# Order of ScalarE's copies and sines, and of VectorE's products, in a gated token mixer

## The reference, cut to what matters

```python
# attention: q, k, v, f_logit are [4, 8, 768, 48]
state = f[:, :, t, :, None] * state + k[t] outer v[t];  y[t] = q[t] @ state
# first mixer: x is [4, 768, 384]
theta = x @ w_theta
zr = x * cos(theta);  zi = x * sin(theta)
y = einsum('ts,bsd->btd', w_tok_r, zr) + einsum('ts,bsd->btd', w_tok_i, zi)
u = x + y
x2 = u + maximum(u @ w_ch, 0)
# second mixer
h = maximum(x2 @ w_in, 0);  u, v = halves of h;  v_n = normalised v
out = (u * (w_spatial @ v_n + b_spatial)) @ w_out
```

## Time and profile before

| | us |
|---|---|
| median of 3 executions | 602.97 |
| lowest, highest | 602.34, 603.02 |
| the profiled execution | 602.97 |
| its span, first to last instruction | 601.0 |
| PE busy | 574.9 (96%) |
| DVE busy | 366.5 (61%) |
| ACT busy | 290.1 (48%) |

### The profile page before, as it was taken

The page is one execution under the profiler, slowest core; times in us unless marked ns, Lnnn a source line. Parts: engine busy times, 40 slices in busy tenths (PEclk is TensorE's granted clock), DMA queues, the critical chain, the costliest instruction groups (busy, mean ns, idle before and its releaser), DMA issues.

```text
span 601.0 us, 11881 instructions
## 1 busy us (share of the span) xinstructions
PE 574.9 (96%) x4226; PEld 554.1 (92%) x4226; DVE 366.5 (61%) x614; ACT 290.1 (48%) x509; POOL 35.9 (6%) x66
## 2 busy tenths in 40 slices
PE   0898999999999999999999999999999999999997
PEld 0787888899999999999999999999999999999996
DVE  6899999777695557446754686556055705570250
ACT  5699999666553334424443536125222522262111
POOL 3223333100000000000000000000000000000000
PEclk9999999999999999999999999999999999999999
DMA  8988989477011230112023550200120010001102
GB/s 169 206 237 255 254 254 301 127 248 253 13 40 41 67 97 35 63 58 75 13 106 104 238 172 2 79 1 1 65 93 1 0 52 26 1 1 40 39 1 81
DMA packets 31113, 58.74 MB, mean 98 GB/s; under 512 B 3680, under 2 KB 23136, under 8 KB 30688
## 3 DMA queue, kind: packets, MB, share of 16 engines
q1 hardware_dynamic: 31072, 58.21, 31.7%
HBM read 44.04 MB, written 14.16 MB: 97 GB/s over the span
## 4 chain that ended last, share of the span: by engine, by line
PE 74%; DVE 3%; issue 2%; ACT 1%; DVEq 0%; ACTq 0%
PE gate_ps L1074 17%; PE theta_bank L1074 11%; PE ringc L1074 11%; PE small_ps L1074 10%; PE mix_ps L1540 8%; PE mix_ps L1545 8%; PE mix_ps L1541 8%; PE small_ps L1504 1%; PE mix_ps L1074 1%; DVE stats L2072 1%; DVE w_lo L79 0%; ACT v L1930 0%; DVE x L1738 0%; DVE vn L2090 0%; ACT w_hi L74 0%
## 5 line engine op out<-in xcount | busy, mean ns | idle before, releaser
L1540 PE MATMUL mix_ps<-w_hi,z_hi 128*128 128x384 f32 x288 | 98.7, 343 | 0.0
L1541 PE MATMUL mix_ps<-w_lo,z_hi 128*128 128x384 f32 x288 | 96.7, 336 | 0.0
L1545 PE MATMUL mix_ps<-w_hi,z_lo 128*128 128x384 f32 x288 | 73.6, 337 | 0.0
L1074 PE MATMUL gate_ps<-w_hi,w_lo 128*128 128x384 f32 x192 | 64.3, 335 | 0.0
L1074 PE MATMUL gate_ps<-w_hi 128*128 128x384 f32 x192 | 64.3, 335 | 0.0
L1074 PE MATMUL gate_ps<-w_lo,w_hi 128*128 128x384 f32 x192 | 64.2, 335 | 0.0
L74 ACT ACTIVATE g_hi<-gate 128x384 fp32r<-128x384 f32 x32 | 16.8, 526 | 81.6 <-DVE gate L2122 81.6
L2118 DVE TENSOR_TENSOR gate<-gate_ps,b_all 128x384 f32<-128x384 f32 x32 | 17.8, 557 | 62.5 <-PE gate_ps L1074 62.5
L1540 PEld LDWEIGHTS mix_ps<-w_hi,z_hi 128*128 128x128 f32 x288 | 54.2, 188 | 0.1
L1541 PEld LDWEIGHTS mix_ps<-w_lo,z_hi 128*128 128x128 f32 x288 | 54.3, 188 | 0.0
L1545 PEld LDWEIGHTS mix_ps<-w_hi,z_lo 128*128 128x128 f32 x288 | 51.9, 188 | 0.3 <-DVE z_lo L79 0.3
(11 more groups left out here) (161 smaller groups left out, 1402.2 us busy)
## 6 DMA issues: line engine op xcount, KB each, us to landing
f_raw<-in_fT_dram SPq DMA_DIRECT2D x32, 144.0 KB, 3.6
k_raw<-in_kT_dram SPq DMA_DIRECT2D x32, 144.0 KB, 3.2
q_raw<-in_qT_dram SPq DMA_DIRECT2D x32, 144.0 KB, 3.8
v_raw<-in_vC_dram SPq DMA_DIRECT2D x16, 288.0 KB, 4.3
xT<-y_sb SPq DMA_DIRECT2D x32, 144.0 KB, 3.5
xt<-xT SPq DMA_DIRECT2D x8, 576.0 KB, 4.1
w_raw<-in_wB_dram SPq DMA_DIRECT2D x6, 768.0 KB, 5.9
u<-xT SPq DMA_DIRECT2D x8, 576.0 KB, 5.0
```

The source lines that it names most:

```text
L1074: done = pe.matmul(out, a, b, start=(first and n == 0), stop=(last and n == len(terms) - 1))
L1540: pe.matmul(out, z, w_hi[:, weights_of[r]], start=(s == 0 and r == 0), stop=False)
L1541: pe.matmul(out, z, w_lo[:, weights_of[r]], start=False, stop=False)
L1545: last = pe.matmul(out, part(z_lo[i], r * DMODEL + d * 128, 128), w_hi[:, weights_of[r]], start=False, stop=(s == ST - 1 and r == 1))
```

## The change

On ACT, `xn_out(1)` of the first batch leaves `first_z` for the head of `rest`, and `xn_out(2)` moves behind `weights_up(1)`. In the list for all batches `xn_out(s+1)` and `trigs(s)` change places for s = 0 to 4; for s = 5 the sines already stood first. On DVE, `multiply(1)` moves ahead of `add_mix(2)` and `add_mix(3)`. The branch that redoes the first piece no longer waits for or makes the second copy.

```diff
-        REDO_Z, REDO_ZHI, REDO_ZLO, REDO_NEXT_TURN, REDO_ALL = 47, 48, 49, 50, 52
+        REDO_Z, REDO_ZHI, REDO_ZLO, REDO_NEXT_TURN, REDO_ALL = 47, 48, 49, 50, 51
...
-            eng.wait_ge(xn_done.h, xn_done.at(FIRST, 2))
...
             def first_z():
                 trigs(0)(FIRST)
-                xn_out(1)(FIRST)
                 z_up(0)(FIRST)
...
-                act.wait_ge(redone, REDO_NEXT_TURN)
-                act.activation(part(xn, DMODEL, DMODEL), small_ps[:, 0:DMODEL], ACT.Copy).then_inc(redone, 1)
...
             def rest(stored):
+                xn_out(1)(FIRST)
                 to_turns(1)(FIRST)
-                xn_out(2)(FIRST)
                 trigs(1)(FIRST)
                 weights_up(1)(FIRST)
+                xn_out(2)(FIRST)
...
-   ... [(xn_out(3), 1), (trigs(2), 1), (weights_up(2), 1), (w_in_up(0), 1),
-   (z_up(2), 1), (to_turns(3), 1), (xn_out(4), 1), (trigs(3), 1), (weights_up(3), 1), (w_in_up(1), 1),
-   (z_up(3), 1), (to_turns(4), 1), (xn_out(5), 1), (trigs(4), 1), (x_hi(0), 0), (weights_up(4), 1), (w_in_up(2), 1),
+   ... [(trigs(2), 1), (xn_out(3), 1), (weights_up(2), 1), (w_in_up(0), 1),
+   (z_up(2), 1), (to_turns(3), 1), (trigs(3), 1), (xn_out(4), 1), (weights_up(3), 1), (w_in_up(1), 1),
+   (z_up(3), 1), (to_turns(4), 1), (trigs(4), 1), (xn_out(5), 1), (x_hi(0), 0), (weights_up(4), 1), (w_in_up(2), 1),
     (z_up(4), 1), (to_turns(5), 1), (trigs(5), 1), (xn_out(0), 0), (weights_up(5), 1), (w_in_up(3), 1),
-   (z_up(5), 1), (to_turns(0), 0), (xn_out(1), 0), (trigs(0), 0),
-   (z_up(0), 0), (to_turns(1), 0), (xn_out(2), 0), (trigs(1), 0), (x_hi(1), 0), (x2_up, 1), ...
+   (z_up(5), 1), (to_turns(0), 0), (trigs(0), 0), (xn_out(1), 0),
+   (z_up(0), 0), (to_turns(1), 0), (trigs(1), 0), (xn_out(2), 0), (x_hi(1), 0), (x2_up, 1), ...
...
-   (z_down(0), 0), (add_mix(0), 1), (add_mix(1), 1), (reduce(1), 0), (x2_down, 1), (add_mix(2), 1), (add_mix(3), 1),
-   (multiply(1), 0), (x_lo(1), 0), (weights_down(1), 0), (add_mix(4), 1), (add_mix(5), 1), (weights_down(6), 1)], 2, 1)
+   (z_down(0), 0), (add_mix(0), 1), (add_mix(1), 1), (reduce(1), 0), (x2_down, 1), (multiply(1), 0), (add_mix(2), 1),
+   (add_mix(3), 1), (x_lo(1), 0), (weights_down(1), 0), (add_mix(4), 1), (add_mix(5), 1), (weights_down(6), 1)], 2, 1)
```

More of the change, by code:

```diff
@@ L1478, in rest @@
                 batches(act, [
-                    (z_up(1), 1), (second_half, 1), (to_turns(2), 1), (u_up(0), 2), (u_up(1), 2)] + [(w_c_up(n), 2) for n in range(WC_PARTS)] + [(xn_out(3), 1), (trigs(2), 1), (weights_up(2), 1), (w_in_up(0), 1),
-                    (z_up(2), 1), (to_turns(3), 1), (xn_out(4), 1), (trigs(3), 1), (weights_up(3), 1), (w_in_up(1), 1),
-                    (z_up(3), 1), (to_turns(4), 1), (xn_out(5), 1), (trigs(4), 1), (x_hi(0), 0), (weights_up(4), 1), (w_in_up(2), 1),
+                    (z_up(1), 1), (second_half, 1), (to_turns(2), 1), (u_up(0), 2), (u_up(1), 2)] + [(w_c_up(n), 2) for n in range(WC_PARTS)] + [(trigs(2), 1), (xn_out(3), 1), (weights_up(2), 1), (w_in_up(0), 1),
+                    (z_up(2), 1), (to_turns(3), 1), (trigs(3), 1), (xn_out(4), 1), (weights_up(3), 1), (w_in_up(1), 1),
+                    (z_up(3), 1), (to_turns(4), 1), (trigs(4), 1), (xn_out(5), 1), (x_hi(0), 0), (weights_up(4), 1), (w_in_up(2), 1),
                     (z_up(4), 1), (to_turns(5), 1), (trigs(5), 1), (xn_out(0), 0), (weights_up(5), 1), (w_in_up(3), 1),
-                    (z_up(5), 1), (to_turns(0), 0), (xn_out(1), 0), (trigs(0), 0),
-                    (z_up(0), 0), (to_turns(1), 0), (xn_out(2), 0), (trigs(1), 0), (x_hi(1), 0), (x2_up, 1), (weights_up(1), 0), (weights_up(6), 1)], 2, 1)
+                    (z_up(5), 1), (to_turns(0), 0), (trigs(0), 0), (xn_out(1), 0),
+                    (z_up(0), 0), (to_turns(1), 0), (trigs(1), 0), (xn_out(2), 0), (x_hi(1), 0), (x2_up, 1), (weights_up(1), 0), (weights_up(6), 1)], 2, 1)
             return {"open": opened, "first_x": first_x, "first_turns": first_turns, "first_z": first_z, "redo": redo, "rest": rest}
```

## The result

The changed kernel takes 608.71 us (median of five, 608.19 to 608.99), the one before 602.49 in the same comparison (602.32 to 603.02). The ratio, which is that of the means and counts eight executions of the changed kernel, is 1.0094, with a 95% interval of 1.0081 to 1.0107: slower, by about 6 us. The forecast was 608.8 us.

What follows compares the result with a forecast made beforehand. PE (TensorE) was taken to be saturated through the mixer, so delays add in full: 3.55 + 1.21 + 1.11 = 5.87 us on 602.97 gives 608.8 us. Range 606.0 to 610.3.

Steps and rivals of the forecast that it cites:

- PE has no hole to make up for a delay: Mixer: PE is saturated from 129 us, so lateness is lost in full; at most 1.3 us can be won.
- Turnover: From attention into the first batch: turn(2) starts at 117.83, +1.41 us at mix(0, 0), 0.2 left after holes close.
- The open 0.37 on DVE: Turnover: to_turns(1) slips 0.37 us; taken as 0 for what follows on DVE, with 0.37 as upper end.
- First batch's chain: ACT and DVE's chain gets three copies, 1.12 us; PE's z_lo product of mix(4, 0) is 0.53 us late.
- multiply(1) ahead of the additions: Second batch, DVE: add_mix(2) ends later, so mix(0, 1) starts at 171.90, a total of 1.55 us late.
- channel(0) and channel(1): PE waits for xn_out copies: channel(0) 2.0 us late in total, channel(1) 3.55 in total, then 1.21 and 1.11 more.
- The swaps priced at nothing: Other copy swaps, such as xn_out(5) before channel(3) with a margin of 1.2 us, were to cost nothing.
- Rival (a): First batch's chain has unseen slack; only channel(1) and 0.2 from the turnover count: +3.5, 606.5 us; chance 0.12.
- (b): Rival: as forecast, but channel(3) or channel(0) wait in later batches as well: +7.4, 610.4 us; chance 0.04.
- (c): Rival: bank emptied in time for channel(1); PE may win its 1.3 us: 601.7 us, faster; chance 0.02.
- (d): Rival: gains and stalls cancel, time 603 us; chance 0.04.

Runs made afterwards that it cites:

- e2: Changed kernel with xn_out(4) put back ahead of trigs(3): ratio to the kernel before 1.0034, length +1.63 us.
- e4: Changed kernel with multiply(1) put back behind add_mix(2) and add_mix(3): ratio to the kernel before 1.0102, length +5.41 us.
- e8: e4 with xn_out(2) also put back ahead of trigs(1): ratio to the kernel before 1.0092, length +4.95 us.
- e1: Kernel before with xn_out(4) alone moved behind trigs(3), in all batches: ratio to the kernel before 1.0067, length +4.29 us.
- e9: Changed kernel with add_channel(0) moved behind reduce(3) in the fourth batch alone: ratio to the kernel before 1.0071, length +4.60 us.
- e6: Changed kernel with add_channel(0) moved behind reduce(3) instead of ahead of z_down(2): ratio to the kernel before 1.0111, length +6.09 us.

## Why the prediction was right

**PE has no hole to make up for a delay.** Right. The last group ends 5.99 us later in the trace, 0.12 of it from attention; this is what PE had lost by channel(1) of the fourth batch (second matmul at 307.37, 301.38 before). Two rows of the kernel before, for this and for the turnover:

```profile
128.39 0.34 PE L1074 MATMUL theta_bank<-w_lo,xt_hi 128*128 128x384 f32 x1
...
301.38 0.34 PE L1074 MATMUL small_ps<-u_lo,w_hi 128*128 128x384 f32 x1
```

The second matmul of each group that waits shows what PE had lost by then. The trace's column is the difference between the kernels' traces, counted from the first `z_hi`:

| lost at | forecast | trace |
|---|---|---|
| turnover, up to theta(3) | 0.20 | 0.27 |
| mix(4, 0), `z_lo`, first batch | 0.33 | 0.30 |
| mix(0, 1), `u`, second batch | 1.02 | 1.02 |
| channel(0), second batch | 0.45 | 0.46 |
| channel(1), second batch | 1.55 | 1.50 |
| channel(1), third batch | 1.21 | 1.17 |
| channel(1), fourth batch | 1.11 | 1.15 |
| sum | 5.87 | 5.87 |

Every term is where it was forecast, within 0.07 us. That the sums agree to 0.01 is luck, as the errors cancel. So is part of 608.8 against 608.71: the forecast started from 602.97, and the kernel before took 602.49 in the comparison. A wait is dearer than its mark: for 1.23 us ahead of channel(1) PE loses 1.50, since the mark begins at the modelled end of the matmul before (0.17 us later than the next could have started), and the first step behind a wait is 0.28 us instead of 0.17.

**Turnover.** Right in mechanism and size: turn(2) at 118.02 - 0.12 = 117.90 (forecast 117.83), the second matmul of theta(3) at 128.77 - 0.12 = 128.65 against 128.39 before, 0.26 late where 0.2 was forecast; alone the edit costs 0.26. The open 0.37 on DVE was 0: reduce(1) starts 2.44 us behind the first `z_hi` against 2.43 before.

**First batch's chain.** Right: the first z_lo product of mix(4, 0) at 151.81 - 0.12 = 151.69, forecast 151.67. It makes about half of the 1.63 that e2 still loses.

**multiply(1) ahead of the additions.** mix(0, 1) starts where it was forecast (172.04 - 0.12 = 171.92, forecast 171.90). What the prediction lacked is that the two additions also hid xn_out(2): it charged 0.94 - 0.11 to them, while about 0.4 of that would have come without them. The sum did not suffer, since next to the additions the copy adds nothing: x_lo(1) follows them without a wait. e4, which takes the additions away, laid the copy open, and e8 took its 0.4 us back.

**channel(0) and channel(1).** 180.52, 188.10, 247.6 and 307.0 were forecast, the last two with the shifts of the steps before; less 0.12 the trace has 180.52, 188.08, 247.54 and 307.00. e1 shows that this swap by itself makes 73% of the loss. e9 shows that the sines are late for channel(1) of the fourth batch because reduce(3) stands behind add_channel(0); in e6 the third batch's wait goes with the same move.

**The swaps priced at nothing.** Right: no wait ahead of channel(3) appears, nor of any turn but turn(2) at the turnover. xn_out(2) is the exception: undone on top of e4 (e8) it gives back 0.46 us, so its price of nothing held only next to the product's move. xn_out(1), xn_out(3) and xn_out(5) were not moved alone in any run. Rival (a) was the nearest; the time of 608.71 against its 606.5 and e2 rule it out. (b) is ruled out by PE's list, (c) and (d) by the time.

The measured medians differ by 6.2 us, the ratio stands for 5.7, and the lengths differ by 5.87; the 0.3 between them are within the spread of attention's part, and no run separates them.

## What to carry to other kernels

When one engine is saturated, read each reordering of the others from its side: what does it wait for, and how far ahead of its need does that end now? A copy that frees a shared bank belongs into the wait that an engine has anyway, ahead of work whose input isn't there yet; put behind that work it inherits all of its lateness (here 4.29 us for one copy of 0.37). And what fills a wait may also cover for a neighbour, so a part taken away alone need not give back what it was charged.

## What the runs showed of the hardware

In e6 PE's granted clock fell after the wait of 2.35 us ahead of turn(4). The table by stretch for PE (length, busy us, granted clock, DMA):

```profile
182.00:185.00 3.00, 0.65 (x5) 1.00 0.00 0
185.00:187.00 2.00, 2.00 (x12) 0.76 0.26 98
187.00:188.00 1.00, 1.00 (x5) 0.50 0.09 16
188.00:190.00 2.00, 2.00 (x9) 0.63 0.00 0
190.00:195.00 5.00, 5.00 (x31) 1.00 0.11 39
```

0.50 is the 1.2 GHz level. From 186.3 to 189.2 us the matmuls start 0.32 us apart instead of 0.174, which at nine or ten of them is another 1.4 us: PE is 2.0 us behind the kernel before ahead of the wait and 6.1 us behind it at 189.5, so the wait cost about 4 us in all. The waits of 1.38 and 1.23 us in the changed kernel and that of 1.52 in e1 left the clock at 1.00. I had not counted on a loss of clock at either length.
